# Attention and two MLPs in one kernel: where the softmax division is done, and how much a half unit turns and multiplies

## What is computed

```python
# attention: q, k, v are (4, 8, 576, 64)
scores = q @ k^T / 8
kth = 32nd largest score of each row
scores = where(scores >= kth, scores, -1e9) - rowmax
attn = exp(scores);  attn = attn / (sum(attn) + 1e-9)
x = (attn @ v) laid out as 2304 tokens x 512
# first MLP: 512 -> 1536 -> 512
y = (sigmoid(x @ w_gate) * (x @ w_val)) @ w_out
# second MLP: 512 -> 2048 -> 512
out = relu(y @ w_in)**2 @ w_out2
```

## Time and profile before

| | |
|---|---|
| median of 3 runs | 1292.53 us (1289.55 to 1294.18) |
| profiled execution, its time | 1294.77 us |
| profiled execution, its span | 1293.0 us |
| PE busy (matmul) | 1227.7 us, 95% |
| PE busy (weight load) | 1017.6 us, 79% |
| DVE busy | 840.3 us, 65% |
| ACT busy | 756.3 us, 58% |
| POOL busy | 502.0 us, 39% |

### The profile page before, as it was taken

The page is one execution under the profiler, slowest core; times in us unless marked ns, Lnnn a source line. Parts: engine busy times, 40 slices in busy tenths (PEclk is TensorE's granted clock), DMA queues, the critical chain, the costliest instruction groups (busy, mean ns, idle before and its releaser), DMA issues.

```text
span 1293.0 us, 22147 instructions
## 1 busy us (share of the span) xinstructions
PE 1227.7 (95%) x7744; PEld 1017.6 (79%) x7744; DVE 840.3 (65%) x1692; ACT 756.3 (58%) x1742; POOL 502.0 (39%) x491
## 2 busy tenths in 40 slices
PE   4679998799999999999999999999999999999999
PEld 2458877578888988888888777777777777888999
DVE  7979998367688956868995757677953433630121
ACT  6887877376668666656765666466644433641221
POOL 4754456255456424323532333234422321430221
PEclk9789999999999999999999999999999999999999
DMA  7866676677575775554566454444455545556997
GB/s 276 303 237 229 191 221 216 215 256 241 173 251 183 261 250 166 183 190 159 176 188 198 159 175 160 160 141 154 163 180 167 199 156 169 175 174 194 350 363 273
DMA packets 89245, 267.52 MB, mean 207 GB/s; under 512 B 9904, under 2 KB 15024, under 8 KB 89136
## 3 DMA queue, kind: packets, MB, share of 16 engines
q1 hardware_dynamic: 89136, 266.12, 61.0%
HBM read 225.71 MB, written 40.37 MB: 206 GB/s over the span
## 4 chain that ended last, share of the span: by engine, by line
PE 84%; DMA 6%; ACT 4%; issue 2%; SPq 1%; DVE 1%; POOL 1%; ACTq 0%; DVEq 0%; POOLq 0%
PE ps L474 22%; PE ps L476 20%; PE ps L475 20%; PE ps L382 6%; PE ps L393 6%; PE ps L409 5%; DMA w_split<-ring 4%; PE ps L460 4%; PE ps L403 1%; PE ps L415 1%; DMA ring<-w_in 1%; ACT below L510 1%; DVE top L634 1%; ACT scores L505 1%; DVE work L636 1%
## 5 line engine op out<-in xcount | busy, mean ns | idle before, releaser
L701 POOL TENSOR_TENSOR below<-scores,below 128x576 f32<-128x576 f32 x144 | 206.3, 1433 | 356.3 <-ACT below L517 356.1
L634 DVE MAX8 top<-work 128x8 f32<-128x576 f32 x432 | 312.9, 752 | 5.0
L474 PE MATMUL ps<-xy_hi,ring 128*128 128x512 f32 (+3 forms) x800 | 297.6, 372 | 1.7 <-POOL xy_lo L725 1.7
L476 PE MATMUL ps<-xy_hi,ring 128*128 128x512 f32 (+3 forms) x800 | 284.0, 355 | 0.0
L475 PE MATMUL ps<-xy_lo,ring 128*128 128x512 f32 (+3 forms) x800 | 283.2, 354 | 0.0
L636 DVE MATCH_REPLACE8 work<-top,work 128x576 f32<-128x576 f32 x288 | 213.8, 742 | 0.0
L474 PE MATMUL ps<-g_hi,ring 128*128 128x512 f32 (+3 forms) x560 | 206.5, 369 | 0.0
L476 PE MATMUL ps<-g_hi,ring 128*128 128x512 f32 (+3 forms) x560 | 198.1, 354 | 0.0
L475 PE MATMUL ps<-g_lo,ring 128*128 128x512 f32 (+3 forms) x560 | 197.5, 353 | 0.0
L474 PEld LDWEIGHTS ps<-xy_hi,ring 128*128 128x128 f32 x800 | 151.5, 189 | 45.4 <-issue 28.7
L661 DVE SCALAR_TENSOR_TENSOR full_buf<-act_buf,ps 128x512 f32<-128x512 f32 (+3 forms) x60 | 35.7, 594 | 213.5 <-PE ps L476 204.5
(11 more groups left out here) (62 smaller groups left out, 1765.8 us busy)
## 6 DMA issues: line engine op xcount, KB each, us to landing
ring<-w_split SPq DMA_DIRECT2D x318, 512.0 KB, 3.6
w_split<-ring SPq DMA_DIRECT2D x68, 512.0 KB, 4.1
ring<-w_in SPq DMA_DIRECT2D x113, 256.0 KB, 3.3
vt<-v_in SPq DMA_DIRECT2D x32, 320.0 KB, 3.2
heads_in<-qk_in SPq DMA_DIRECT2D x16, 336.0 KB, 4.5
heads_in<-qk_in SPq DMA_DIRECT2D x16, 240.0 KB, 3.7
heads_in<-qk_in SPq DMA_DIRECT2D x8, 368.0 KB, 5.3
heads_in<-qk_in SPq DMA_DIRECT2D x8, 304.0 KB, 4.0
```

Of the source, the lines that this page charges most:

```text
L474: nc.tensor.matmul(dst, w_hi, hi[:, k, 0:WIDTH[c]], start=first, stop=False)
L476: mm = nc.tensor.matmul(dst, w_lo, hi[:, k, 0:WIDTH[c]], start=False, stop=final)
L634: nc.vector.max(out=best, in_=sc if step == 0 else wk).then_inc(sel_step[t % 2], 1)
L701: nc.gpsimd.tensor_tensor(out=below[:, t % 2, :], in0=scores[:, t % 4, :], in1=below[:, t % 2, :], op=ALU.subtract).then_inc(mask_done, 1)
```

## The change

- Normalisation moves from x to the probabilities. For each tile, ACT adds 1e-9 to the row sum, DVE inverts it, and POOL multiplies the tile of 128x576 probabilities by it in place (new `normalise`, one slot after the exponential). The spread inverses (L415), `copy_pv` and the multiplications on x go. ACT copies the product straight into x (`copy_x`), in the slot of the products.
- The products with v of the last 64 keys are two products with 64 columns of weights side by side.
- A half unit has its probabilities in one row of 576 (head 1 with its keys rolled by 64, as they were loaded), so one exponential, five transposes and two copies do. Its products have 64 columns; for them v has a third part of 320 more columns, rolled by 64 keys, which is loaded only for pairs with an odd number of blocks (960 columns instead of 640).
- Order: NORM is 3, TURN stays 3 but the turn is the last thing PE does in the slot, and the products with v are one slot later (PROD, 4). MLP_AT becomes 16, 40, 68, 100, 132, 148. `split_x` comes at the earliest five slots after a pair's last tile, before four. `pe_ns` has new figures, so `shares` deals differently. On ACT the weight splits follow the exponential, before they stood ahead of `copy_pt`; on DVE `invert` comes early in the slot; on POOL the evacuations come before `split_x`.

```diff
-VCOLS = 2 * KFULL * DH + P
+VTAIL = KFULL * DH
+VSECOND = VTAIL + P
+VROLLED = VSECOND + KFULL * DH
+VCOLS = VROLLED + (KFULL + 1) * DH
...
-MASK, TURN, NORM = 2, 3, 4
-MLP_AT = [CHUNK_END[c] + (4 if c in (0, NC - 1) else 5) for c in range(NC)]
+MASK, NORM, TURN, PROD = 2, 3, 3, 4
+MLP_AT = [CHUNK_END[c] + 5 for c in range(NC)]
...
-    t, u = s + 2, UNIT_AT.get(s - TURN)
-    score = 0 if t >= NT else 1070 if TILES[t][1] == 2 else 535
-    return score + (0 if u is None else 2400)
+    t, u, v = s + 2, UNIT_AT.get(s - TURN), UNIT_AT.get(s - PROD)
+    turned = 0 if u is None else 550 if UNITS[u][4] else 980
+    products = 0 if v is None else 800 if UNITS[v][4] else 1300
+    return (800 if t < NT else 0) + turned + products
...
-        _s = max(END[X_UNIT[_c][_p]] + NORM, slot_of_block(_c - 1, OUT0 - 1) + 1)
+        _s = max(END[X_UNIT[_c][_p]] + PROD + 1, slot_of_block(_c - 1, OUT0 - 1) + 1)
...
             def turn(u):
-                pe.wait_ge(exp_done, END[u] + 1)
+                pe.wait_ge(norm_done, END[u] + 1)
                 wait(pe, pt_copied, u)
-                wait(pe, pv_copied, u)
...
+                wait(pe, x_done, u)
+                half = UNITS[u][4]
...
-                for k in range(NBLK):
+                for k in range(KFULL + 1 if half else NBLK):
...
             def times_v(u):
-                nc.tensor.matmul(ps[:, RR, PV:PV + P], vt[:, g % 2, KFULL * DH:KFULL * DH + P],
-                                 pt[:, u % 2, P * KFULL:P * KFULL + P], start=True, stop=False)
-                for k in range(KFULL):
+                n = B64 if half else P
+                for k in range(KFULL + 1):
                     for h in range(2):
...
+                        if half:
+                            v_at, p_at = (VROLLED if h else 0) + DH * k, P * k + B64 * h
+                        elif k < KFULL:
+                            v_at, p_at = VSECOND * h + DH * k, P * ((KFULL + 1) * h + k)
+                        else:
+                            v_at, p_at = VTAIL + DH * h, P * KFULL
...
-                pe.wait_ge(inv_done, u + 1)
-                for h in range(2):
-                    m = 0 if UNITS[u][4] else h
-                    mm = nc.tensor.matmul(ps[DH * h:DH * h + DH, RR, 0:P], rinv[:, u % 2, m:m + 1].to_broadcast([P, DH]),
-                                          ident[:, :], start=True, stop=True)
...
             for s in range(SLOTS):
-                u = UNIT_AT.get(s - TURN)
-                if u is not None:
-                    turn(u)
...
-                if u is not None:
-                    times_v(u)
+                if s - PROD in UNIT_AT:
+                    times_v(UNIT_AT[s - PROD])
                 for c, h in SHARES[s][2]:
                     mlp_half(c, h)
+                if s - TURN in UNIT_AT:
+                    turn(UNIT_AT[s - TURN])
...
-            def copy_pv(u):
-                act.wait_ge(pv_done, u + 1)
-                wait(act, x_done, u - 1)
-                nc.scalar.activation(rp[:, u % 2, :], ps[:, RR, 0:PV + P], ACT.Copy).then_inc(pv_copied, 1)
+            def copy_x(u):
+                c, g, p, i, half, col = UNITS[u]
+                act.wait_ge(pv_done, u + 1)
+                if c > 1:
+
+                    act.wait_ge(x_lo_done, (c - 2) * NM + p + 1)
+                x, n = (x0 if c == 0 else xf), (B64 if half else P)
+                nc.scalar.activation(x[:, p, col:col + n], ps[:, LAST, PV:PV + n], ACT.Copy).then_inc(x_done, 1)
...
+            def normalise(t):
+                pool.wait_ge(inv_done, t + 1)
+                nc.gpsimd.tensor_tensor(out=probs_of(t), in0=probs_of(t),
+                                        in1=rinv[:, t % 4:t % 4 + 1].to_broadcast([P, SEQ]),
+                                        op=ALU.mult).then_inc(norm_done, 1)
```

More of the change, by code:

```diff
@@ L223, in qk_of, with probs_of @@
             return qk[at:at + P * cols].rearrange("(p c) -> p c", p=P)
-        def probs_of(u):
-            return probs_h[:, :, :] if UNITS[u][4] else probs[:, RANK[u] % 2, :, :]
+        def probs_of(t):
+            u, part = TILES[t]
+            return probs_h[:, 0:SEQ] if part == 2 else probs[:, RANK[u] % 2, part, :]
         def place(k):
@@ L606, in _ @@
                     evac(c, n)
-                if s - NORM in UNIT_AT:
-                    copy_pv(UNIT_AT[s - NORM])
-                for k in SPLIT_AT.get(s, []):
-                    split_weights(k)
-                if s - TURN in UNIT_AT:
-                    copy_pt(UNIT_AT[s - TURN])
+                if s - PROD in UNIT_AT:
+                    copy_pt(UNIT_AT[s - PROD])
                 for c, p in X_AT.get(s, []):
@@ L616, in _ @@
                     exp(s - MASK)
+                for k in SPLIT_AT.get(s, []):
+                    split_weights(k)
                 for c, n in blocks_of(SHARES[s][0] + SHARES[s][1]):
                     evac(c, n)
+                if s - PROD in UNIT_AT:
+                    copy_x(UNIT_AT[s - PROD])
             for c, n in blocks_of(SHARES[SLOTS - 1][2]) + blocks_of(REST):
@@ L644, in select_both, with invert @@
                         select(s, step)
-            def invert(u):
-                heads = 1 if UNITS[u][4] else 2
-                dve.wait_ge(sum_done, u + 1)
-                wait(dve, pv_done, u - 1)
-                nc.vector.reciprocal(rinv[:, u % 2, 0:heads], rsum_eps[:, u % 2, 0:heads]).then_inc(inv_done, 1)
+            def invert(t):
+                dve.wait_ge(sum_done, t + 1)
+                wait(dve, norm_done, t - 3)
+                nc.vector.reciprocal(rinv[:, t % 4:t % 4 + 1], rsum_eps[:, t % 4:t % 4 + 1]).then_inc(inv_done, 1)
             def evac(c, n):
@@ L795 @@
     v_in = v.reshape(heads // 2, 2, SEQ, DH)
-    full = v_in[:, :, :KFULL * P].reshape(heads // 2, 2, KFULL, P, DH).transpose(0, 1, 3, 2, 4)
-    full = full.reshape(heads // 2, 2, P, KFULL * DH)
+    rolled = np.zeros((heads // 2, (KFULL + 1) * P, DH), np.float32)
+    rolled[:, :SEQ] = np.roll(v_in[:, 1], B64, axis=1)
     tail = np.zeros((heads // 2, 2, B64, 2, DH), np.float32)
@@ L800, with by_block @@
         tail[:, h, :, h] = v_in[:, h, KFULL * P:]
-    v_a = np.concatenate([full[:, 0], tail.reshape(heads // 2, P, P), full[:, 1]], axis=2)
+    def by_block(a):
+        return a.reshape(heads // 2, -1, P, DH).transpose(0, 2, 1, 3).reshape(heads // 2, P, -1)
+    v_a = np.concatenate([by_block(v_in[:, 0, :KFULL * P]), tail.reshape(heads // 2, P, P),
+                          by_block(v_in[:, 1, :KFULL * P]), by_block(rolled)], axis=2)
     source = {"gate": moe_w_gate, "val": moe_w_val, "y": moe_w_out, "h": moe2_w_in, "out": moe2_w_out}
```

95 lines of the change are left out of this document (36 added, 59 removed).

## The result

| | before | after |
|---|---|---|
| median of the runs | 1293.36 us (1289.55 to 1294.65, 4 runs) | 1274.04 us (1271.13 to 1277.31, 4 runs) |
| ratio, 95% interval | | 0.9856 (0.9823 to 0.9889) |
| profiled execution: time, span | 1294.77, 1293.0 us | 1273.17, 1271.4 us |

What follows compares the result with a forecast made beforehand. TensorE was taken as the bound from 275 us on. Units -21.4, up to 275 us +1.0, chunk starts +6.8 and the last wait -1.7 sum to -15.3 us, a median of 1277 us; range 1264 to 1294.

Steps and rivals of the forecast that it cites:

- The bound: From 275 to 1150 us TensorE is busy 871.4 of 875.0 us, so work it sheds comes off one for one.
- Full units: TensorE's products of a full unit fall from 1.55 to 1.32 us, saving 0.23 us in each of 46 units.
- Half units: Turns, spread and 64-column products of a half unit save TensorE 0.90 us, between 0.63 and 1.17, in 12 units.
- Rival 4: Half units' products: 64 columns cost as 128 (weight loads), -18.2 instead of -21.4 us, 1280; inside the forecast, no own chance.
- Sum of the units: TensorE's saving after 275 us: 10.6 us from full and 10.8 from half units, 21.4 us, 18.2 to 24.6.
- GpSimd: The new 128x576 multiplication takes 1.4 us, 144 times, hidden behind GpSimd's waits for ScalarE.
- First stretch: Before chunk 0's MLP: ScalarE's slot takes 5.8 us, and the MLP starts 2.5 us later.
- Chunk starts: At chunks 2, 3 and 4 TensorE waits for the last pair's split of x: 2.6, 1.2, 3.0, in all +6.8 us.
- The last wait: The last chunk's 1.7 us wait for the split of x goes, as three half blocks stand between: -1.7 us.
- Rival 1: No waits at chunk starts, and columns alone price the half units: -26 us, 1266; chance 0.17.
- Rival 2: ScalarE and TensorE wait for each other from 87 to 275 us, chunk starts cost 11: -2 us, 1290.4; chance 0.2.
- Rival 3: copy_x couples ScalarE to the products, 0.5 us lost in each of 58 units after 275 us: +29, 1306; chance 0.13.

Runs made afterwards that it cites:

- splitting first: The changed kernel with the split of x moved ahead in its slot, behind ScalarE's score copy and first on GpSimd: 1260.63 us, ratio 0.9758.
- the three parts undone: Three runs, each the changed kernel with one part undone: spread products back 1284.02 us, nine turns per half unit 1277.89 us, half-unit products with 128 columns 1279.77 us.
- the doubled one: The changed kernel with each tile's normalisation on GpSimd done twice, first into a spare buffer: 1299.14 us, ratio 1.0051.
- the last experiment: The kernel with x split first, with GpSimd's normalisation of a tile ahead of the next tile's mask instead of behind it: 1278.04 us, ratio 0.9887.

## Why the prediction was right, and where it wasn't

- **The bound.** Right. What TensorE no longer does after 275 us comes off one for one. Stretch by stretch with 0.23 and 1.18 us a unit: chunk 1's MLP has 12 full and 4 half units, 7.5 us, less 0.3 of idle time, measured 7.1. Chunk 2's has 16 full, 3.7, less 3.7 for wait, restart and clock, measured 0.0. Chunks 3 and 4 have 20 full and 8 half, 14.0, less 0.7 of idle time (2.96 of new waits in place of 2.24 before) and 0.5 of restarts (the 3.5 us that splitting first got back there, less 2.96 of waits), measured 12.6.
- **Full units.** 0.23 forecast, 0.23 measured. The products themselves got 0.31 shorter; the forecast's two changes of form are there, one of them in the record ahead. The Trainium skill (TensorEngine Tiling (Array Packing), "Key Properties") says that changing the tiling mode drains TensorE, with no price; the 0.08 to 0.10 us per change that move about here and never vanish agree.
- **Half units: the term that was mis-sized.** 0.90 forecast as the middle of 0.63 and 1.17, 1.18 measured, 12 x 0.28 = 3.4 us. The measured value lies just outside the bounds. I had split the difference between "only columns count" and "weight loads set the pace" where nothing in the trace spoke for the second. Ten pairs take 0.73 us, with a change of form, and the run with 128 columns gives the 6.5 us back. Rival 4 is out. The turn was a little better too, 0.44 for 0.40.
- **Sum of the units.** 46 x 0.23 + 12 x 1.18 = 24.7 us, against 21.4 forecast and 21.8 (or 25.4, see above) for the three parts undone.
- **GpSimd.** Forecast 1.4, measured 1.20 us on average, x144, with a median of 1.15. I took the end of the bracket at L701; the one at L750, 1.24 by elements, was the nearer: an operand that is one value a partition costs no more than a tile read twice. The Trainium skill's figure (GPSIMD Engine Reference, "Performance versus the Vector engine", an estimated 1.25 us) agrees with the run better than my row did; its rule that such work belongs on VectorE ("When to use GPSIMD") doesn't change the sign here, since one normalisation is hidden. That it is hidden "behind its waits for ScalarE" was right but thinner than I wrote: the doubled one cost 25 us, and the turned order 17. The guess that GpSimd's work slows L672 on VectorE holds as well: the nine single records of 512 columns, before and after, in whose time GpSimd does nothing take 0.67 to 0.69 us, the others up to 1.72. The mean went from 1.02 to 1.05 us (L676 after the change), and TensorE waited for none of them.
- **First stretch.** Right. The first MLP product came at 89.63 us, 2.4 later (forecast 2.5). VectorE's slots took 5.14 us at first and 5.6 to 5.8 from slot 11 on, when its lead was used up and ScalarE's pace, 5.6 to 5.8 from the start, held it (forecast 5.8). I called that pace ScalarE's own. It is that of the ring of ScalarE and GpSimd in the last experiment: the 2.21 us from L517 to L527 in my sum hold a wait for the mask, and the mask stands behind GpSimd's weight splits. Up to the start of chunk 1's MLP it came to -0.9 us; the 2 us allowed for waits there weren't needed (TensorE's idle time in chunk 0's MLP fell from 8.7 to 5.7 us; in the second profile of the changed kernel it is 7.4).
- **Chunk starts.** The mechanism and places were right, to the slot, and the order of their sizes: 2.6, 1.2 and 3.0 us forecast, 1.96, 0.51 and 2.45 measured. From `copy_x` at 457.62 to the end of the split at 463.44 are 5.8 us for my 6.3, by the cheaper normalisation and split. But each wait costs 0.3 us of restart besides, and behind the one of 2 us the clock stayed low for over 3 us and cost 1.5; the sum had no line for either. The errors nearly cancel: 6.8 forecast, against 4.9 of waits and 2.2 behind them. That is luck: the clock did not fall at chunk 4, where the second profile of the changed kernel has it fall. In slot 40 the idle time hardly grew (12.3 to 12.6 us), as forecast, but one wait of 11.1 us took the place of two of 4.6 and 4.7, and splitting first showed that 4.5 of it could be had.
- **The last wait** of 1.7 us fell to 0.72, not to 0.
- **Rivals.** Rival 1 was right on the price of columns and wrong on the waits. Rival 2 fell: the stretch from 90 to 240 us got shorter. Rival 3 fell: ScalarE does wait for the products in 59 slots, 126.2 us, but of what stands behind TensorE waits after 300 us only for two score copies, 1.07 us, and for the split at chunk starts; the slack held.

So -15.3 was the sum of gains forecast 3.3 us too small and of costs that were about right by errors against each other. Between the profiled spans, 21.6 us, the forecast is 6.3 short: 3.3 for the units, 1.9 for the first two stretches, and 2.2 of waits during the MLPs of chunks 3 and 4 before the change (two turns for `copy_pv`, one spread product for its inverse), which went and stood in no sum; 0.4 more at chunk starts and 0.8 less gained at the last wait go the other way. What stays open is TensorE's last 8.1 us of idle time in chunk 1's MLP. Of the changes of order, only the deal of the half blocks and the places of `split_x`, `copy_x` and `normalise` were tested by themselves; the turn at the end of the slot, the products a slot later and the early `invert` were not.

## What to carry to other kernels

Before a step is put "somewhere in the slot" of an in-order queue, write down who waits for what stands behind it: one small split moved to the front of two queues was worth 12 us, two thirds of what the whole change brought (7 of them the change had itself cost), and one operation moved ahead of its neighbour cost 17. A share of 0.5 on a helper engine says nothing of whether another microsecond fits; look for the wait in which it would lie, and at its length. And price a wait on TensorE, where it is the bound, above its own length: by 0.3 us for the restart here, and by some 1.5 us more where the clock fell, which it did behind 8 of 14 waits of about 2 us.

## What the runs showed of the hardware

- Products of 64 columns, side by side in the two halves of the array, cost by their columns: ten pairs 0.73 us from start to start, with 128 columns 1.24 (each with 0.08 for a change of form).
- The change between 128 and 64 columns of weights costs 0.08 to 0.10 us, and it shows in the distance behind the last record of the old form. Whoever adds up a new form from its own records misses it.
- A wait of 1.96 us in a stream at 2.4 GHz was followed by some 3.4 us at 1.2 GHz (448-column records 0.37 us apart instead of 0.20), worth 1.5 us. In the version without the wait the same stretch runs at 1.00 throughout and is 3.7 us shorter. But with the last keys' product wide, the same wait of 1.96 us left the clock at 2.4 GHz; over all profiles it fell behind 8 of 14 waits of 1.9 to 2.5 us.
- A restart behind a wait costs TensorE 0.3 us beyond the wait: 2.32 us from start to start for a wait of 1.96, and 0.31 instead of 0.20 us to the next start.
- On GpSimd a 128x576 multiplication by one value a partition takes 1.20 us on average (median 1.15), a subtraction of two full tiles (L706, x144) 1.42.
